# The opening of a three-layer kernel: another order of all queues, with more of the weight preparation on GpSimd

## The chip, the cores and the metric

One core of one Trainium2 chip runs the whole program. The metric is the device time of one execution in microseconds (us); a figure without more is the median of several executions. The engines are TensorE (PE) for matrix products, VectorE (DVE), ScalarE (ACT), GpSimd (POOL), and SyncE (SP), which here issues the DMAs. They run side by side, each through its own queue of instructions in a fixed order, and meet at semaphores.

## What is computed

Attention over a window of 128 positions, whose result goes through two feed-forward layers:

```python
# _attn_ref: batch 4, 8 heads, 576 positions, head size 64
scores = scale * np.matmul(q, k.transpose(0, 1, 3, 2))
bias = slopes[:, None, None] * (-np.abs(rel).astype(np.float32))[None, :, :]
mask = (rel >= 0) & (rel < window)
scores = np.where(mask, scores + bias[None], -1000000000.0)
attn = np.exp(scores - max); attn = attn / (sum + 1e-09)
x = np.matmul(attn, v)                       # 2304 tokens x 512
# _moe_ref: 512 -> 1024 -> 512
h = x @ w_in
solu = h * softmax(h)
ln = (solu - mu) / np.sqrt(var + 1e-06) * g_ln
x = ln @ w_out
# _moe2_ref: 512 -> 1536 -> 512
g = x @ w_gate
out = (g * (1.0 / (1.0 + np.exp(-g))) * (x @ w_val)) @ w_out2
```

All in float32. The large products split each factor into a high and a low part and run three fast passes: high x high, high x low, low x high.

## The kernel before

**Tiles.** The 2304 tokens are 18 tiles of 128. For each tile t the heads come in two groups g of four. The first two layers are one loop over the tiles (`step`), three stages deep; the third layer (`period`, `out_product`) follows and is not touched. Tiles 0 to 2 and the scores of tile 3 have their own, hand-written order in each of the five queues: the functions `opening()`. After them every queue goes on with `step(3)`, whose first work on PE is `qk_scores(4, 0)` (L558).

**A tile's way.** SP loads keys and queries (`load_early` for tiles 1 to 3, `load_qk` from 4 on) and v. PE makes scores (`early_scores(a, g)`, L545). ACT copies the half that belongs to the previous tile's keys into `fold` (`copy_prev`), DVE puts the own half over it (`select_own`, L1120) and finds the maxima (`find_max`). ACT takes the exponentials (`exp_scores`, L837 and L840), DVE inverts the sums (`invert_sums`, L1134), and POOL scales `fold` (`scale_probs`, L1467; DVE does it for tile 0). PE transposes (`transpose_probs`, L567), DVE masks (`unfold`, L1153), PE multiplies with v (`attend`, L582). ACT and DVE split the result (`x_hi_part`, `x_lo_part`). PE makes the hidden layer in two halves n of four chunks c (`hidden(t, n, odd, chunks)`, L596). DVE finds its maximum (`max_hidden`), ACT the exponentials (`exp_hidden`), DVE the product and the statistics (`make_solu`, `find_stats`, `scale_variance`), POOL the factor (`find_factor`, L1472 to L1478), ACT normalises. PE transposes (`transpose_ln`, L609), ACT and DVE split (`ln_hi`, `ln_lo`). `layer1_out` (L623) multiplies with w_out for two tiles at a time.

**The weight pieces.** Eight pieces of 128x1024 (512 KB) go through four buffers `stage`: pieces 0 to 3 are w_in (chunk c of `hidden(0, 0)` waits for the low part of piece c), pieces 4 to 7 are w_out. `load_piece(n)` for n of 4 and more waits for the low part of piece n - 4. A piece is split in two steps: the high part is a copy (ACT, L813), the low part a difference (`piece` on POOL, L1506 for w_in and L1512 for w_out, or on DVE, L1205). The rows of w_out are also scaled by the norm weights g_ln first, in two instructions of 512 columns: on ACT (L889) for pieces 4, 6 and 7, on POOL (`gain_piece`, L1461) for piece 5, as `POOL_GAINS` says. Before, the low parts of w_in are POOL's for pieces 0 and 1 and DVE's for 2 and 3. POOL also makes the low parts of the keys (`split_last_k`, L1445, for tile 3, and `split_qk`, L1434 and L1437, two instructions for each group) and copies rows of positions (`put_positions`, L1451).

**Fillers.** `keep_warm(n)` (L524) issues n products of 128x128 whose result nobody reads.

**Order.** Nothing reorders the queues: a queue whose head waits holds all behind it. `scores_ready`, `x_ready`, `probs_ready` and so on count the units done, so `wait_ge(scores_ready, 2 * (t - 1) + g + 1)` in `load_early` holds SP, and all loads behind, until PE has made the scores that free the buffer.

## Time and profile before

| | us |
|---|---|
| median of 3 runs | 721.79 (721.65 to 722.07) |
| the profiled execution | 720.79 |
| its span, first to last instruction | 719.0 |

Busy shares of the span: PE 99%, DVE 67%, ACT 57%, POOL 54%. The profile page splits the span into 40 slices and shows for each the busy tenths of the engines and the TensorE clock that was granted. The trace behind it is asked in views: the waits (who waited for whom), the timeline (instructions in order of time, equal ones in a row merged), groups of instructions by line and form, and DMA issues with the time to landing. In a row, `banks` is PSUM, `out<-in` names the tiles, and L with a number is a line of the kernel. The end of a matrix product is modelled, its start is measured.

### The profile page before, as it was taken

The page shows a single profiled execution, that of the slowest core. Times are in us where ns is not written, and L with a number is a line of the kernel's source. Part 1 is how long each engine was busy: PE and PEld are TensorE (multiplying, and loading weights), DVE is VectorE, ACT ScalarE, POOL GpSimd, SP SyncE. Part 2 cuts the span into 40 slices and gives each one's busy share as a digit, 9 for nine tenths or more (in the row PEclk, how much of TensorE's full clock was granted, in tenths as well). Part 3 has the DMA queues.
Part 4 walks back from the last instruction along what each step waited for, and adds up shares of the span by engine and source line. Part 5 has one row for each costly group of instructions (what it writes and reads, how often), then busy time and mean ns, then how long its engine had stood idle before and what let it go on. Part 6 is the DMA issues. An engine that isn't in the chain of part 4 may idle for free.

```text
span 719.0 us, 13230 instructions
## 1 busy us (share of the span) xinstructions
PE 711.5 (99%) x4732; PEld 682.6 (95%) x4732; DVE 482.4 (67%) x851; ACT 412.3 (57%) x843; POOL 390.3 (54%) x398
## 2 busy tenths in 40 slices
PE   8999999999999999999999999999999999999998
PEld 7779999999999999999999999999999999999998
DVE  5987777777777777747976555655556699754650
ACT  6997777777777776673634443344433487245340
POOL 3785444444445555894838958769576937300000
PEclk9999999999999999999999999999999999999999
DMA  8734443333333323134223432414336765795822
GB/s 326 285 104 162 166 143 120 129 134 128 117 117 117 117 73 118 33 115 132 84 101 135 153 107 107 150 64 154 107 107 242 256 234 190 274 375 191 283 75 88
DMA packets 49197, 109.85 MB, mean 153 GB/s; under 512 B 3841, under 2 KB 30209, under 8 KB 49153
## 3 DMA queue, kind: packets, MB, share of 16 engines
q1 hardware_dynamic: 49152, 109.27, 43.5%
q8 instruction: 27, 0.44, 0.2%
q14 instruction: 18, 0.14, 0.1%
HBM read 75.04 MB, written 34.21 MB: 152 GB/s over the span
## 4 chain that ended last, share of the span: by engine, by line
PE 95%; DVE 2%; DMA 2%; issue 0%; SPq 0%; ACT 0%; DVEq 0%
PE banks L637 36%; PE banks L795 18%; PE banks L623 15%; PE banks L596 13%; PE banks L582 4%; PE banks L609 2%; PE banks L567 2%; PE banks L558 2%; PE banks L559 2%; DMA early<-in_early 1%; DMA v<-in_v 1%; PE banks L545 1%; DVE win_lo L1205 0%; DVE xs_lo L1213 0%; DVE fold L1120 0%
## 5 line engine op out<-in xcount | busy, mean ns | idle before, releaser
L637 PE MATMUL banks<-xs_hi,w_hi 128*128 128x384 f32 x504 | 169.5, 336 | 0.1
L637 PE MATMUL banks<-xs_hi,w_lo 128*128 128x384 f32 x504 | 169.3, 336 | 0.0
L637 PE MATMUL banks<-xs_lo,w_hi 128*128 128x384 f32 x504 | 169.1, 336 | 0.0
L637 PEld LDWEIGHTS banks<-xs_hi,w_hi 128*128 128x128 f32 x504 | 94.7, 188 | 0.7 <-DVE xs_lo L1213 0.4
L637 PEld LDWEIGHTS banks<-xs_lo,w_hi 128*128 128x128 f32 x504 | 94.7, 188 | 0.0
L637 PEld LDWEIGHTS banks<-xs_hi,w_lo 128*128 128x128 f32 x504 | 94.7, 188 | 0.0
L623 PE MATMUL banks<-lnt_hi,wout_hi 128*128 (+1 forms) x288 | 85.5, 297 | 0.0
L795 PE MATMUL banks<-lot_hi,wo_hi 128*128 128x384 f32 x252 | 84.8, 337 | 0.1
L795 PE MATMUL banks<-lot_hi,wo_lo 128*128 128x384 f32 x252 | 84.5, 335 | 0.0
L795 PE MATMUL banks<-lot_lo,wo_hi 128*128 128x384 f32 x252 | 84.4, 335 | 0.0
L813 ACT ACTIVATE g_sum<-banks 128x384 f32<-128x384 f32 x84 | 41.2, 490 | 72.1 <-PE banks L637 55.9
L623 PE MATMUL banks<-lnt_lo,wout_hi 128*128 (+1 forms) x288 | 81.4, 283 | 0.0
L623 PE MATMUL banks<-lnt_hi,wout_lo 128*128 (+1 forms) x288 | 81.4, 283 | 0.0
L1236 DVE TENSOR_TENSOR lot_lo<-lot_raw,lot_hi 128x768 fp32r<-128x768 f32 x63 | 61.7, 1036 | 22.4 <-ACT lot_hi L813 22.4
L1434 POOL TENSOR_TENSOR k_lo<-qk_raw,kq 64x512 fp32r<-64x512 f32 x28 | 36.0, 1286 | 58.9 <-ACT kq L813 58.9
L1522 POOL TENSOR_TENSOR w_raw<-w_raw 128x256 f32<-128x256 f32 x48 | 41.1, 856 | 46.4 <-DMA w_raw<-in_wb 43.5
L1549 POOL TENSOR_TENSOR w_lo<-w_raw,w_hi 128x256 fp32r<-128x256 f32 x77 | 65.3, 883 | 0.8 <-ACT w_hi L813 0.8
L1467 POOL TENSOR_TENSOR fold<-fold,pinv 128x512 f32<-128x512 f32 x34 | 35.4, 1042 | 44.0 <-DVE pinv L1136 44.0
L596 PE MATMUL banks<-win_hi,xt_hi 128*128 128x512 f32 x144 | 56.9, 395 | 1.2 <-DVE xt_lo L1160 1.1
L813 ACT ACTIVATE lot_hi<-lot_raw 128x768 fp32r<-128x768 f32 x63 | 48.1, 834 | 17.4 <-DMA lot_raw<-unit_scratch 17.4
L1241 DVE TENSOR_TENSOR g_sum<-banks,g_sum 128x384 f32<-128x384 f32 x42 | 23.3, 556 | 51.1 <-PE banks L637 45.2
L623 PEld LDWEIGHTS banks<-lnt_hi,wout_hi 128*128 128x128 f32 x288 | 55.0, 191 | 2.6 <-issue 2.6
(106 smaller groups left out, 1751.5 us busy)
## 6 DMA issues: line engine op xcount, KB each, us to landing
lot_raw<-unit_scratch SPq DMA_DIRECT2D x63, 384.0 KB, 5.6
qk_raw<-in_qk SPq DMA_DIRECT2D x28, 768.0 KB, 4.2
unit_scratch<-st_sums SPq DMA_DIRECT2D x18, 576.0 KB, 4.7
unit_scratch<-st_even SPq DMA_DIRECT2D x18, 384.0 KB, 2.5
unit_scratch<-st_odd SPq DMA_DIRECT2D x18, 384.0 KB, 3.2
w_raw<-in_wb SPq DMA_DIRECT2D x12, 512.0 KB, 4.6
v<-in_v SPq DMA_DIRECT2D x18, 256.0 KB, 2.6
x_scratch<-x_out SPq DMA_DIRECT2D x18, 256.0 KB, 2.6
```

What stands on the lines that cost most here:

```text
L582: last = mm(ps_x[HD * half:HD * (half + 1), c * P:(c + 1) * P], v[:, of_v, head * HD:(head + 1) * HD], of_p[:, g, 2 * pair + half, :], sta ...
L596: last = mm(ps_h[:, n, :], xt[l][:, odd, c, :], win[r][:, c, n * 512:(n + 1) * 512], start=c == 0 and k == 0, stop=c == CM - 1 and k == 2)
L623: last = mm(ps, wout1[l][:, c, f * P:(f + 1) * P], lnt[r][:, gx % 2, c, :], start=c == 0 and n == 0, stop=c == C1 - 1 and n == 2)
L637: last = mm(ps[n % 2], w_of[l][:, k * P:(k + 1) * P], x_of[r][:, k * HALF:(k + 1) * HALF], start=start and k == 0 and i == 0, stop=k == 1 ...
L795: last = mm(ps[p], w_of[l][:, c, p * P:(p + 1) * P], lot_parts[lot % RING][r][:, cols], start=start and c == 0 and i == 0, stop=c == CHUNK ...
L813: return nc.scalar.activation(out, in_, ACT.Copy)
L1236: nc.vector.tensor_tensor(lo[:, :], lot_raw[k % RING][:, :], hi[:, :], ALU.subtract).then_inc(lot_done, 1)
L1241: nc.vector.tensor_tensor(g_sum[n % 2][:, 1, :], ps_c[n % 2], g_sum[n % 2][:, 1, :], ALU.add).then_inc(gates_done, 1)
L1434: nc.gpsimd.tensor_tensor(k_lo[k, g, :, odd, :], qk_raw[k, g, :, 2 * odd, :], kq[k, g, :, 3 * odd, :], ALU.subtract).then_inc(k_lo_done, 1)
L1467: nc.gpsimd.tensor_tensor(fold[:, g, :, :], fold[:, g, :, :], inv, ALU.mult).then_inc(probs_ready, 1)
L1522: last = nc.gpsimd.tensor_tensor(out[:, cols], one[:, cols], two[:, cols], op)
L1549: last = nc.gpsimd.tensor_tensor(w_parts[b][1][:, slot, :], w_raw[b][:, slot, :], w_parts[b][0][:, slot - 1, :], ALU.subtract)
```

## The change

Only the openings change, and what they need:

- POOL makes the high part of piece 1 (`piece_hi`, with a semaphore of its own, `win_hi_pool`), which was ACT's. `win_hi_of(n)` says whose semaphore counts piece n.
- The low parts of w_in: DVE takes pieces 0 and 2, POOL 1 and 3.
- POOL scales pieces 6 and 7 instead of 5, ACT 4 and 5 instead of 4, 6 and 7.
- `keep_warm(2)` ahead of `transpose_probs(0, 0)`, and 6 instead of 4 fillers ahead of `attend(0, 0)`.
- All five queues have another order. On SP, `early(2,0)` stands ahead of v(0), the last keys of tile 3 ahead of piece 2; v(1) is earlier, piece 7 and `qk(4,1)` later. On PE, `early_scores(2, 1)` and `(3, 0)` are earlier, `(3, 1)` is behind `attend(2, 0)`, and `hidden` is cut so that transposes come in between.

The diff, without most of its unchanged lines:

```diff
--- before.py
+++ after.py
@@ -73,7 +73,7 @@
...
 E_MASK, E_SLOTS = 8, 17
-POOL_GAINS = (5,)
+POOL_GAINS = (6, 7,)
 ACT_GAINS = tuple(n for n in range(CM, 8) if n not in POOL_GAINS)
@@ -193,6 +193,7 @@
...
         warm_set = sem("warm_set")
+        win_hi_pool = sem("win_hi_pool")
         win_hi, win_lo_pool, win_lo_dve = sem("win_hi"), sem("win_lo_pool"), sem("win_lo_dve")
@@ -262,9 +263,14 @@
...
+        def win_hi_of(n):
+
+            pool_takes = (1,)
+            return (win_hi_pool if n in pool_takes else win_hi), 1 + sum((m in pool_takes) == (n in pool_takes) for m in range(n))
+
         def win_lo(n):
-            return (win_lo_pool, win_lo_pool, win_lo_dve, win_lo_dve)[n], (1, 2, 1, 2)[n]
+            return (win_lo_dve, win_lo_pool, win_lo_dve, win_lo_pool)[n], (1, 1, 2, 2)[n]
@@ -361,24 +367,24 @@
...
                 load_piece(1)
+                load_early(2, 0)
                 load_v(0, 0)
-                load_piece(2)
-                load_early(2, 0)
-                load_piece(3)
-                load_piece(4)
-                load_early(2, 1)
-                load_piece(5)
                 for g in range(2):
                     load_last_k(g)
+                load_piece(2)
+                load_piece(3)
+                load_early(2, 1)
+                load_v(1, 1)
+                load_piece(4)
+                load_early(3, 0)
+                load_piece(5)
                 load_piece(6)
-                load_v(1, 1)
-                load_early(3, 0)
-                load_piece(7)
                 load_early(3, 1)
...
                 load_v(2, 0)
+                load_piece(7)
+                load_v(3, 1)
                 load_qk(4, 1)
-                load_v(3, 1)
                 for g in range(2):
@@ -725,33 +731,41 @@
...
                 pe.wait_ge(const_in, 16)
+                keep_warm(2)
                 transpose_probs(0, 0)
...
                 transpose_probs(0, 1)
-                keep_warm(4)
+                keep_warm(6)
                 attend(0, 0)
...
                 transpose_probs(1, 0)
-                hidden(0, 0, 0, range(1, CM))
-                hidden(0, 1, 0)
+                hidden(0, 0, 0, range(1, 3))
+                early_scores(2, 1)
+                hidden(0, 0, 0, range(3, CM))
+                hidden(0, 1, 0, range(0, 1))
                 transpose_probs(1, 1)
-                early_scores(2, 1)
+                hidden(0, 1, 0, range(1, CM))
                 attend(1, 1)
+                early_scores(3, 0)
                 transpose_probs(2, 0)
-                early_scores(3, 0)
                 hidden(1, 0, 1)
-                hidden(1, 1, 1)
+                hidden(1, 1, 1, range(0, 2))
+                transpose_probs(2, 1)
+                hidden(1, 1, 1, range(2, CM))
                 transpose_ln(0, 0, 0)
-                transpose_probs(2, 1)
+                attend(2, 0)
                 early_scores(3, 1)
-                attend(2, 0)
+                hidden(2, 0, 0, range(0, 1))
+                hidden(2, 0, 0, range(1, 3))
                 transpose_ln(0, 1, 0)
-                hidden(2, 0, 0)
+                hidden(2, 0, 0, range(3, CM))
+                hidden(2, 1, 0, range(0, 1))
                 transpose_probs(3, 0)
+                hidden(2, 1, 0, range(1, 2))
                 transpose_ln(1, 0, 1)
-                hidden(2, 1, 0)
+                hidden(2, 1, 0, range(2, CM))
                 transpose_ln(1, 1, 1)
@@ -996,35 +1010,34 @@
...
                 exp_scores(0, 1)
+                copy_prev(1, 0, 1)
                 piece(0)
-                copy_prev(1, 0, 1)
-                piece(1)
                 copy_prev(1, 1, 1)
...
                 piece(3)
+                copy_prev(2, 0, 0)
                 exp_scores(1, 1)
-                copy_prev(2, 0, 0)
-                piece(4)
                 exp_scores(2, 0)
                 split_last_k(0)
+                split_last_k(1)
                 copy_prev(2, 1, 0)
+                piece(4)
                 exp_hidden(0, 0)
-                piece(5)
                 x_hi_part(1, 1)
                 exp_scores(2, 1)
+                piece(5)
                 copy_prev(3, 0, 1)
-                split_last_k(1)
                 piece(6)
...
                 split_qk(4, 0, 0)
+                ln_hi(0, 0, 0, 0)
                 exp_hidden(1, 1)
-                ln_hi(0, 0, 0, 0)
+                x_hi_part(2, 0)
+                piece(7)
                 exp_scores(3, 0)
                 copy_prev(3, 1, 1)
-                x_hi_part(2, 0)
-                piece(7)
                 ln_hi(0, 1, 0, 0)
@@ -1201,7 +1214,7 @@
...
-                dve.wait_ge(win_hi, n + 1)
+                dve.wait_ge(*win_hi_of(n))
                 nc.vector.tensor_tensor(win[1][:, n, :], stage[:, n % STAGES, :], win[0][:, n, :],
@@ -1322,43 +1335,43 @@
...
                 select_own(1, 1, 1)
-                find_max(1, 1)
+                piece(0)
                 invert_sums(1, 0)
                 x_lo_part(0, 0)
+                find_max(1, 1)
                 piece(2)
-                piece(3)
-                invert_sums(1, 1)
                 select_own(2, 0, 0)
                 find_max(2, 0)
+                invert_sums(1, 1)
                 unfold(1, 0)
+                invert_sums(2, 0)
                 max_hidden(0, 0, 0)
                 unfold(1, 1)
+                select_own(2, 1, 0)
                 max_hidden(0, 1, 0)
-                invert_sums(2, 0)
-                select_own(2, 1, 0)
                 find_max(2, 1)
...
                 find_stats(0, 0)
+                invert_sums(2, 1)
                 scale_variance(0, 0)
-                invert_sums(2, 1)
+                unfold(2, 0)
                 select_own(3, 0, 1)
-                unfold(2, 0)
                 max_hidden(1, 0, 1)
+                unfold(2, 1)
+                max_hidden(1, 1, 1)
                 find_max(3, 0)
-                max_hidden(1, 1, 1)
-                unfold(2, 1)
+                ln_lo(0, 0, 0, 0)
                 make_solu(1, 1)
-                ln_lo(0, 0, 0, 0)
+                x_lo_part(2, 0)
                 find_stats(1, 1)
-                x_lo_part(2, 0)
                 scale_variance(1, 1)
...
                 find_max(3, 1)
+                max_hidden(2, 0, 0)
                 ln_lo(0, 1, 0, 0)
                 unfold(3, 0)
-                max_hidden(2, 0, 0)
                 invert_sums(3, 1)
@@ -1461,6 +1474,11 @@
...
+            def piece_hi(n):
+                pool.wait_ge(stage_in[n % STAGES], 16)
+                nc.gpsimd.tensor_copy(win[0][:, n, :], stage[:, n % STAGES, :]).then_inc(win_hi_pool, 1)
+                pool.wait_ge(*win_hi_of(n))
+
             def scale_probs(t, g):
@@ -1502,7 +1520,7 @@
...
                 if n < CM:
-                    pool.wait_ge(win_hi, n + 1)
+                    pool.wait_ge(*win_hi_of(n))
                     nc.gpsimd.tensor_tensor(win[1][:, n, :], src, win[0][:, n, :],
@@ -1582,26 +1600,28 @@
...
                 pool.wait_ge(const_in, 16)
-                piece(0)
+                piece_hi(1)
                 piece(1)
                 scale_probs(1, 0)
+                piece(3)
                 scale_probs(1, 1)
-                gain_piece(5)
-                pool.wait_ge(probs_ready, 4)
-                put_positions(0)
                 scale_probs(2, 0)
                 split_last_k(0)
+                pool.wait_ge(probs_ready, 5)
+                put_positions(0)
+                split_last_k(1)
+                gain_piece(6)
                 piece(4)
+                scale_probs(2, 1)
                 find_factor(0, 0)
-                scale_probs(2, 1)
+                gain_piece(7)
+                piece(5)
+                split_qk(4, 0, 0)
                 pool.wait_ge(probs_ready, 6)
                 put_positions(1)
-                piece(5)
-                split_last_k(1)
-                piece(6)
                 find_factor(1, 1)
                 scale_probs(3, 0)
-                split_qk(4, 0, 0)
+                piece(6)
                 scale_probs(3, 1)
...
                 split_qk(4, 1, 0)
```

## Rows read from the trace of the kernel before

**Rows 1.** page, parts 1 and 2: busy time, granted TensorE clock by slices

```profile
PE 711.5 (99%) x4732; PEld 682.6 (95%) x4732; DVE 482.4 (67%) x851; ACT 412.3 (57%) x843; POOL 390.3 (54%) x398
...
PEclk9999999999999999999999999999999999999999
```

**Rows 2.** waits of PE in 0 to 60 us: us in total, times, longest

```profile
PE banks L545 <- DMA early<-in_early: 1.6, 2, 1.2
PE banks L596 <- DVE xt_lo L1160: 1.1, 1, 1.1
```

**Rows 3.** timeline of PE: start us, duration, line, operation, [idle before, releaser]

```profile
13.66 1.06 PE L524 MATMUL banks<-solu 128*128 128x128 f32 x8
14.65 0.66 PE L582 MATMUL banks<-p_own,v 128*64 128x128 f32 x8
...
18.59 0.47 PE L596 MATMUL banks<-win_hi,xt_hi 128*128 128x512 f32 x1 [0.15 <-issue]
...
46.16 0.60 PE L567 MATMUL banks<-const,fold 128*128 128x128 f32 x4
...
50.63 0.36 PE L558 MATMUL banks<-kq 128*128 128x256 f32 x1
```

**Rows 4.** timeline of SP's issues: start us, duration of issuing

```profile
4.15 0.51 SPq L346 DMA_DIRECT2D v<-in_v  x1
4.71 0.95 SPq L351 DMA_DIRECT2D stage<-in_wa  x1
11.25 0.33 SPq L329 DMA_DIRECT2D early<-in_early  x1
...
18.07 1.54 SPq L338 DMA_DIRECT2D qk_raw<-in_qk  x2
```

**Rows 5.** DMA issues near 4.2, 4.7, 15.8, 18.1, 41.7 us; last: to landing

```profile
v<-in_v SPq DMA_DIRECT2D x1, 256.0 KB, 9.5
...
stage<-in_wa SPq DMA_DIRECT2D x1, 512.0 KB, 10.3
...
stage<-in_wa SPq DMA_DIRECT2D x1, 512.0 KB, 5.3
...
qk_raw<-in_qk SPq DMA_DIRECT2D x1, 256.0 KB, 6.0
...
v<-in_v SPq DMA_DIRECT2D x1, 256.0 KB, 3.4
```

**Rows 6.** timeline of ACT

```profile
17.11 1.99 ACT L813 ACTIVATE win_hi<-stage 128x1024 fp32r<-128x1024 f32 x2
...
23.59 0.19 ACT L837 ACTIVATE scaled<-negmax 128x4 f32<-128x4 f32 x1
...
25.36 0.62 ACT L813 ACTIVATE kq<-qk_raw 128x512 fp32r<-128x512 f32 x1
```

**Rows 7.** timeline of POOL

```profile
28.16 1.04 POOL L1467 TENSOR_TENSOR fold<-fold,pinv 128x512 f32<-128x512 f32 x1 [0.39 <-DVE pinv L1136]
...
43.76 0.56 POOL L1472 TENSOR_TENSOR rstd<-var,const 128x1 f32<-128x1 f32 x1 [1.11 <-DVE var L1194]
...
44.81 1.04 POOL L1467 TENSOR_TENSOR fold<-fold,pinv 128x512 f32<-128x512 f32 x1
```

**Rows 8.** POOL by form, 0 to 54 us: busy us, mean ns, idle before

```profile
L1512 POOL TENSOR_TENSOR wout_lo<-stage,wout_hi 128x1024 fp32r<-128x1024 f32 x4 | 9.5, 2382 | 0.2
L1467 POOL TENSOR_TENSOR fold<-fold,pinv 128x512 f32<-128x512 f32 x6 | 6.3, 1042 | 3.9 <-DVE pinv L1136 3.9
...
L1461 POOL TENSOR_SCALAR stage<-stage,const 128x512 f32<-128x512 f32 x2 | 3.1, 1571 | 0.9 <-DMA stage<-in_wa 0.8
L1437 POOL TENSOR_TENSOR kq<-qk_raw,kq 64x512 fp32r<-64x512 f32 x2 | 2.6, 1302 | 0.2
...
L1445 POOL TENSOR_TENSOR k_lo<-qk_raw,kq 64x512 fp32r<-64x512 f32 x2 | 2.6, 1283 | 0.0
L1451 POOL CAST k_lo<-const 64x1024 fp32r<-64x1024 f32 x2 | 2.1, 1038 | 0.1
```

## The prediction

> **What bounds the kernel now.** I read the page first: TensorE (PE) is busy nearly all of the span, and its granted clock is full in all 40 slices [rows 1]. Then the waits of PE. In the first 60 us the largest sums are 1.6 us for `early` tiles and 1.1 us for `xt_lo` [rows 2]; the same view of 54 to 719 us has no line. So behind the opening PE never waits, and the change, which touches only the opening, can do one thing: move the moment at which PE starts `qk_scores(4, 0)`, the first work of the loop, now at 50.63 us [rows 3]. Whatever it moves, the end moves by as much. Therefore the third view is the timeline of PE in the opening (what starts when), and then those of SP's issues, of ScalarE (ACT) and of GpSimd (POOL), since these set when PE may start.
>
> PE itself does the same products before and after, plus four fillers. The sum is thus: new start of the loop = old start + fillers that don't fall into a wait + waits added - waits removed. For the waits I walked the five queues of the opening in their written order, old and new, with the durations of the trace: each operation starts when its engine is free and what it waits for is done.
>
> **Fillers.** Two are added ahead of `transpose_probs(0, 0)`, two more ahead of `attend(0, 0)`. Four took 13.66 to 14.65 us [rows 3], 0.25 us each, so 1.0 us for four. The first two delay the transposes and with them the chain on VectorE (DVE) by 0.5 us at most; the other two fall into a wait that the change itself makes (next part). All 1.0 us delays `attend(0, 0)` only if v is there.
>
> **The loads.** Before, v(0) and piece 2 are issued at 4.15 and 4.71 us, ahead of `early(2,0)`, which waits for scores and goes out at 11.25 [rows 4]; they land 9.5 and 10.3 us later, at 13.65 and 15.0 [rows 5]. After, `early(2,0)` stands in front of both, so SP holds v(0) until 11.25 + 0.4 = 11.6 us, and behind it come both last-k loads, then pieces 2 and 3. From an empty queue v of 256 KB took 3.4 us [rows 5]. The pieces queued one behind the other land some 1.3 us apart for 512 KB (the 256 KB of v 0.7 us), so the fixed part is 3.4 - 0.7 = 2.7 us. Walked on: `early(2,0)` 15.2, v(0) 15.9, last k 16.6 and 17.3, piece 2 18.7, piece 3 20.0 us. The nearest row that speaks for later is a piece issued around 16 us that took 5.3 us [rows 5], 1.3 us more than 2.7 + 1.3; it is the upper bound. The lower one is that all land as before.
>
> **What hangs on them.** `attend(0, 0)` starts at 14.65 now, after at 15.95 (0.9 us from the fillers and their start, 0.4 us waiting for v), and `hidden(0, 0)` at 18.7 in the walk, hardly later than the 18.59 of now [rows 3], since ACT and DVE are then free for the split. ACT splits pieces 2 and 3 from 17.11 in one go, at 1.0 us each [rows 6]; after, it has them only at 18.7 and 20.0, so it leaves piece 3 at 21.0. Behind the waiting `piece(3)` on ACT stand `copy_prev(2, 0)`, `exp_scores(1, 1)` and `exp_scores(2, 0)`. The copy costs 0.5 us, an `exp_scores` 1.8 us (23.59 to 25.36 [rows 6]), so `exp_scores(2, 0)` ends at 25.1 and `invert_sums(2, 0)` lets POOL scale at 25.6 us. (Before this is at 28.16 [rows 7], late because DVE does `invert_sums(2, 0)` behind `unfold(1, 1)` and `max_hidden(0, 1)`; that is a real gain of the new order, 2.5 us for POOL.) PE's waits from this part: 0.8 us for the low part of piece 2 ahead of chunk 2 of `hidden(0, 0)` (0.5 us before, ahead of chunk 3), 0.4 us at `early_scores(2, 1)`, which needs `select_own(2, 0)` and so that copy.
>
> **POOL.** ACT gives up the high part of piece 1 (1.0 us) and a net one of its three scalings (1.3 us). ACT isn't last, so this buys nothing by itself. POOL gets the high part, a cast of 128x1024. The trace has only a cast of 64x1024 at 1.04 us [rows 8]; by lanes it could be anything from that to double; I take 1.04, the same elements per partition. It lies ahead of 18 us, where POOL then waits 1.4 us for `inv_ready`, so at up to double it costs nothing; with less cover it costs itself. The second scaling counts: POOL scales two pieces where it scaled one, 2 x 1.57 us more [rows 8], and between `scale_probs(2, 0)` and `scale_probs(3, 0)` it now does: 3 `scale_probs` 3.1, 2 `split_last_k` 2.6, 2 `put_positions` 2.1, 4 scaling instructions 6.3, 2 low parts of w_out 4.8, `split_qk(4, 0)` 2.6, 2 `find_factor` 2.1 (43.76 to 44.81 [rows 7]): 23.6 us, with gaps of some hundredths 23.8. All inputs are there in time, so it runs from 25.6 to 49.4 without a pause. Before, the scaling of piece 5 lay ahead of `scale_probs(2, 0)`, in a stretch where POOL had been waiting, and `scale_probs(3, 0)` ended at 45.85 [rows 7].
>
> The Trainium skill, "GPSIMD Engine Reference" (4.1, engine selection), says otherwise of such an instruction: with one tensor as input GpSimd runs at roughly line rate, and only two inputs make it slow. The cast, which has one input, shows what that would be: 1024 elements in 1.04 us, so a scaling instruction of 512 in 0.52 us and four of them 4.2 us less. For the scaling the trace doesn't agree: 1.57 us, more than the 1.04 us of the two-input product of the same size [rows 8]. The row decides, and what the rule would give is rival 1.
>
> **PE behind POOL.** `transpose_probs(3, 0)` waits for `scale_probs(3, 0)`; it starts at 46.16 now [rows 3] and 49.5 after. Other waits on POOL's delays: `transpose_probs(2, 1)` 0.7 (scaling of piece 6 and a low part stand ahead of its `scale_probs`), `transpose_ln(0, 0)` 0.5 (`find_factor(0, 0)` ends at 38.0, was 34.4), and `hidden(2, 0)` 0.8 where it was 1.1 [rows 2]. `transpose_probs(3, 0)` itself waits 1.5. From there to the loop: its own 0.44, three chunks of `hidden(2, 1)` at 0.69, two `transpose_ln` and `transpose_probs(3, 1)` at 0.44, 0.3 waiting: 4.1 us (4.5 now, with one chunk more). So the loop starts at 53.6.
>
> Waits after, in sum: 0.4 + 0.8 + 0.4 + 0.2 + 0.7 + 0.5 + 0.8 + 1.5 + 0.3 = 5.6 us, against 3.0 us of the same walk through the old order, plus 1.0 us of fillers: 3.6 us. The walk through the old order gives 50.05 us for the loop's start where the trace has 50.63, so the difference to the trace is 3.0 us. I take the middle, **3.3 us slower**. Of SP's moves only one more matters: `qk(4,1)` now stands behind v(3), which waits for `attend(2, 0)`; issued at 42.3 instead of 40.2 it lands near 47, and ACT wants it at 51.9: no cost.
>
> The profiled execution took 720.8 us (span 719.0), the median of the runs is 721.8, 1.0 us more. So 720.8 + 3.3 = 724.1 profiled, 725.1 as a median. Bounds of this case: loads landing as before take 1.3 us off (2.0 slower, 723.8), landing 1.3 us later adds 1.1, and the gap of 0.3 on either side: up to 4.8 slower, 726.6.
>
> **Rivals.**
> 1. POOL doesn't decide. For: only two scaling instructions stand in the trace [rows 8], side by side, and spans on POOL are rough. If all four ran at the rate of the cast, 0.52 us each, `scale_probs(3, 0)` would end near 45.5, the low parts and `find_factor` would come in time, and the walk gives 2.9 us less (not 4.2, as 0.4 us stays at `transpose_probs(3, 0)`, behind ACT and DVE): 0.4 slower, 722.2, within what can be told from no change. Against: these two instructions started 1.6 us apart. 0.14.
> 2. Faster: the waits shown are what the new order takes away. The 1.1 us ahead of `hidden(2, 0)` goes since `attend(2, 0)`, `early_scores(3, 1)` and the ln transpose are spread, and the 2.5 us that POOL starts earlier outweigh the scaling. All 3.0 us of waits gone less 1.0 us of fillers: 719.8. It decides if piece 3 lands before 18 us and POOL is through with `scale_probs(3, 0)` by 45 us, that is in 20 us where the rows sum to 23.6. 0.08.
> 3. The loads collide worse: v(0), last k and both pieces, now issued within 2.5 us, share the 16 engines instead of following one another (a 256 KB load of last k amid others took 6.0 us where v alone took 3.4 [rows 5]), so that v lands near 18 and piece 3 near 22: 2 us on top, 727.1. 0.06.
> The forecast keeps 0.72.
>
> **How the numbers follow.** A measurement of this kernel can tell about 0.2%, 1.4 us, from no change: faster is below 720.4, slower above 723.2. Slower: 0.72 + 0.06, less a little for the low edge of the main case and rival 1 spilling both ways: 0.77. Same: 0.15. Faster: 0.08. The range goes from rival 1 (722.2) to 727.0, between the upper bound and rival 3; outside are rival 2, half of rival 3 and some of rival 1.
>
> **What would show each step.** v(0) issued at 11.6 and landing near 16, piece 3 landing near 20; ACT idle ahead of `win_hi` twice around 18 to 20 us; four `TENSOR_SCALAR` on POOL at 1.57 us each after 30 us; POOL without a pause from 25.6 to 49; PE waiting for POOL's `fold` ahead of `transpose_probs(2, 1)` and (3, 0), the latter starting at 49.5; PE's first `kq` product near 53.6 instead of 50.63; no waits behind it. I am wrong if POOL has pauses ahead of 45 us, or if pieces land at their old times.

## The result and the profile after

| | before | after |
|---|---|---|
| median, us | 721.25 (720.17 to 722.07, 6 runs) | 725.33 (724.09 to 725.62, 6 runs) |
| the profiled execution, us | 720.79 | 724.99 |
| its span, us | 719.0 | 723.2 |
| first `kq` product of PE (start of the loop), us | 50.63 | 54.82 |

The ratio is 1.0057, 95% interval 1.0045 to 1.0068: 4.1 us slower. Of some 140 executions behind all the ratios below, two are left out: one of e2 that took 742.05 us at a mean granted clock of 0.914, and one of e5 that took 2501.95 us. All of it lies ahead of the loop: from the loop's first product to the end of the span it is 668.4 us in both.

The waits of PE in the first 60 us, after (us in total, times, longest), against [rows 2]:

```profile
PE banks L573 <- DVE p_prev L1167: 1.4, 1, 1.4
PE banks L573 <- POOL fold L1485: 1.3, 1, 1.3
PE banks L588 <- DMA v<-in_v: 1.1, 1, 1.1
...
PE banks L551 <- DMA early<-in_early: 0.7, 1, 0.7
PE banks L551 <- DVE fold L1133: 0.4, 1, 0.4
PE banks L602 <- DVE win_lo L1218: 0.4, 1, 0.4
PE banks L602 <- DVE xt_lo L1173: 0.3, 1, 0.3
...
PE banks L615 <- DVE lnt_lo L1212: 0.2, 1, 0.2
```

Six of them are new: for v (L588), for two `transpose_probs` (L573), for `select_own` (L551, the `fold` line), and two short ones, for the low part of piece 2 (`win_lo`) and for `lnt_lo`. The 1.1 us for `xt_lo` of [rows 2] has shrunk to 0.3. Where they lie, in PE's timeline, against [rows 3]:

```profile
13.68 1.50 PE L530 MATMUL banks<-solu 128*128 128x128 f32 x12
16.33 1.09 PE L588 MATMUL banks<-p_own,v 128*64 128x128 f32 x16 [1.15 <-DMA v<-in_v]
...
19.00 0.58 PE L602 MATMUL banks<-win_hi,xt_hi 128*128 128x512 f32 x1
...
38.64 0.63 PE L573 MATMUL banks<-const,fold 128*128 128x128 f32 x4 [1.38 <-DVE p_prev L1167]
...
50.65 0.65 PE L573 MATMUL banks<-const,fold 128*128 128x128 f32 x4 [1.28 <-POOL fold L1485]
...
54.82 0.36 PE L564 MATMUL banks<-kq 128*128 128x256 f32 x1
```

The loads that come late, as the issues show them (near 11.3, 13.1 and 13.6 us; last: us to landing), against [rows 5]:

```profile
v<-in_v SPq DMA_DIRECT2D x1, 256.0 KB, 5.1
...
stage<-in_wa SPq DMA_DIRECT2D x1, 512.0 KB, 6.1
...
stage<-in_wa SPq DMA_DIRECT2D x1, 512.0 KB, 6.7
```

v(0) lands at 16.3, piece 2 at 19.1 and piece 3 at 20.4 us. ScalarE sits idle for both pieces, and `copy_prev(2, 0)` comes behind them, against [rows 6]:

```profile
19.19 1.06 ACT L827 ACTIVATE win_hi<-stage 128x1024 fp32r<-128x1024 f32 x1 [1.12 <-DMA stage<-in_wa]
20.47 1.06 ACT L827 ACTIVATE win_hi<-stage 128x1024 fp32r<-128x1024 f32 x1 [0.22 <-DMA stage<-in_wa]
21.43 0.58 ACT L827 ACTIVATE fold<-banks 128x512 f32<-128x512 f32 x1
```

POOL's cast of piece 1, and then POOL from `scale_probs(2, 0)` to `scale_probs(3, 0)`, against [rows 7] (the work on keys and positions from 27.06 to 30.90 and from 44.66 to 48.48 and the small instructions of `find_factor` are left out):

```profile
12.69 1.32 POOL L1479 CAST win_hi<-stage 128x1024 fp32r<-128x1024 f32 x1 [11.01 <-DMA stage<-in_wa]
...
26.06 1.04 POOL L1485 TENSOR_TENSOR fold<-fold,pinv 128x512 f32<-128x512 f32 x1 [0.73 <-DVE pinv L1149]
...
30.90 3.23 POOL L1474 TENSOR_SCALAR stage<-stage,const 128x512 f32<-128x512 f32 x2
34.21 2.41 POOL L1530 TENSOR_TENSOR wout_lo<-stage,wout_hi 128x1024 fp32r<-128x1024 f32 x1
36.94 1.04 POOL L1485 TENSOR_TENSOR fold<-fold,pinv 128x512 f32<-128x512 f32 x1 [0.32 <-DVE pinv L1149]
...
39.02 3.23 POOL L1474 TENSOR_SCALAR stage<-stage,const 128x512 f32<-128x512 f32 x2
42.33 2.37 POOL L1530 TENSOR_TENSOR wout_lo<-stage,wout_hi 128x1024 fp32r<-128x1024 f32 x1
...
49.55 1.04 POOL L1485 TENSOR_TENSOR fold<-fold,pinv 128x512 f32<-128x512 f32 x1
```

One pause of 0.32 us in 24.5 us. `transpose_probs(3, 0)` starts at 50.65, right behind it.

### The profile page after: what moved, and what is told of

It is laid out like the page before. It is cut to its first block, busy times and chain, and to the rows that moved or that the text cites. A ratio compares the mean times of both kernels' runs of the same rounds, so it can differ in the third digit from the quotient of the medians.

```text
span 723.2 us, 13248 instructions
## 1 busy us (share of the span) xinstructions
PE 713.1 (99%) x4740; PEld 683.7 (95%) x4740; DVE 483.4 (67%) x851; ACT 410.5 (57%) x840; POOL 394.4 (55%) x401
## 3 DMA queue, kind: packets, MB, share of 16 engines
HBM read 75.04 MB, written 34.21 MB: 151 GB/s over the span
## 4 chain that ended last, share of the span: by engine, by line
PE 92%; DMA 2%; DVE 2%; POOL 2%; ACT 1%; issue 1%; SPq 0%; POOLq 0%; DVEq 0%; ACTq 0%
PE banks L643 36%; PE banks L809 18%; PE banks L629 15%; PE banks L602 12%; PE banks L588 4%; PE banks L615 2%; PE banks L564 2%; PE banks L565 2%; PE banks L573 2%; DMA early<-in_early 1%; DMA stage<-in_wa 1%; PE banks L551 1%; POOL stage L1474 0%; DVE pden L1147 0%; POOL wout_lo L1530 0%
```

## The experiments

All ratios are to the kernel before, on the same chip in the same session; the sessions ran on several chips, and the intervals of two changed kernels often overlap, so a difference between two of them below some 1.4 us is not clear of noise by the ratios alone. e7 and e8 are one execution each, read for their profiles. "Loop" is the start of PE's first `kq` product in the profiled execution (50.63 before, 54.82 after). From there to the end each took 668.3 to 668.6 us (only e11 took 669.0, with one wait of 0.5 us behind the opening), so the loop's start and the time tell the same, apart from how a single execution's first loads land (some tenths, in two cases over a microsecond).

| run | edit | ratio (95%) | loop, us |
|---|---|---|---|
| after | | 1.0057 (1.0045 to 1.0068) | 54.82 |
| e1_scale_one_piece | POOL scales only piece 7 | 1.0027 (1.0016 to 1.0038) | 53.02 |
| e2_loads_early | v(0), pieces 2 and 3 early | 1.0040 (1.0024 to 1.0056) | 53.39 |
| e3_no_extra_fillers | without the four fillers | 1.0064 (1.0045 to 1.0083) | 54.02 |
| e4_add_by_columns | one addition as four | 1.0050 (1.0033 to 1.0067) | 53.97 |
| e5_both_undone | e1, e2 and e3 together | 1.0017 (1.0007 to 1.0026) | 52.31 |
| e10_high_part_on_act | cast back on ACT | 1.0047 (1.0031 to 1.0063) | 54.75 |
| e7_add_128x4_amid_pool | the addition put amid POOL's work | one execution, 725.2 us | 55.02 |
| e8_columns_amid_pool | the same, by columns | one execution, 723.9 us | 53.68 |
| e6_before_late_loads | before, SP order of after | 1.0042 (1.0026 to 1.0057) | 54.20 |
| e12_late_loads_8_fillers | e6 with four fillers more | 1.0035 (1.0023 to 1.0048) | 53.38 |
| e9_before_two_scalings | before, POOL scales 5 and 7 | 1.0029 (1.0017 to 1.0041) | 54.82 |
| e11_before_add_columns | before, one addition as four | 0.9989 (0.9978 to 0.9999) | 50.49 |

**The theories.** The prediction's: POOL has one scaling too many between `scale_probs(2, 0)` and `scale_probs(3, 0)`, and the late loads start that stretch late. Rivals: only one of the two matters; the fillers do; the order of the other queues does.

**POOL's scaling.**

```diff
-POOL_GAINS = (6, 7,)
+POOL_GAINS = (7,)
...
-                gain_piece(6)
                 piece(4)
```

> The changed kernel with GpSimd scaling only piece 7; ScalarE scales piece 6 (one POOL scaling, 3.2 us, less ahead of scale_probs(2, 1)). Theory (POOL decides the opening): scale_probs(3, 0) on POOL starts about 2 us earlier (49.55 in the changed kernel), the loop's first qk product at about 52.9 us instead of 54.82, time 1.9 us below the changed kernel. Rival (the late loads decide, POOL only fills waits): the first qk product stays within 0.4 us of 54.8. Second rival (ScalarE takes POOL's place as the last): under 1 us gained.

The loop starts at 53.02, `scale_probs(3, 0)` on POOL at 47.74. The time falls from 1.0057 to 1.0027, about 2.2 us. The two waits for POOL and for what follows it are gone from PE (L573 0.2 us in all), so ScalarE did not take POOL's place. VectorE did, in part: of the 3.3 us taken from POOL's work 1.8 came through at `scale_probs(3, 0)`, since POOL now stands 1.44 us for `pinv` ahead of `scale_probs(2, 1)` and 0.41 us for `var` ahead of `find_factor(1, 1)`. From the other side, the old kernel with the scaling of piece 7 on POOL as well:

```diff
-POOL_GAINS = (5,)
+POOL_GAINS = (5, 7)
...
                 put_positions(1)
+                gain_piece(7)
                 piece(5)
```

> The kernel before with one part of the change alone: GpSimd also scales piece 7 (behind the second put_positions, ahead of the low part of piece 5), ScalarE is relieved of it. Theory (POOL is near its limit in the opening even in the old order): POOL's scale_probs(3, 0) starts at about 47.0 instead of 44.81, transpose_probs(3, 0) waits 1.9 us for it, and the first qk product is at 52.5, 1.9 us slower. Rival (POOL's 6 us of idle time in the opening take it): under 0.5 us slower.

1.0029, 2.1 us slower, and PE waits 1.9 us for `fold`, once, as expected. The waits of PE in 0 to 60 us:

```profile
PE banks L545 <- DMA early<-in_early: 2.3, 2, 1.4
PE banks L567 <- POOL fold L1467: 1.9, 1, 1.9
```

The profiled execution was the slowest of the six (725.04, median 723.10), and its loop starts at 54.82 instead of the 52.5 expected. PE's timeline behind the wait shows most of it:

```profile
48.75 0.66 PE L567 MATMUL banks<-const,fold 128*128 128x128 f32 x4 [1.91 <-POOL fold L1467]
...
50.36 0.63 PE L596 MATMUL banks<-win_hi,xt_lo 128*128 128x512 f32 x1
50.79 0.63 PE L596 MATMUL banks<-win_hi,xt_hi 128*128 128x512 f32 x1
...
53.34 0.40 PE L596 MATMUL banks<-win_hi,xt_hi 128*128 128x512 f32 x1
53.57 0.40 PE L596 MATMUL banks<-win_lo,xt_hi 128*128 128x512 f32 x1
```

and the granted clock by stretches of 5 us (columns: PE busy, number, granted clock, DMA share, GB/s):

```profile
45.00:50.00 5.00, 3.09 (x18) 0.99 0.61 210
50.00:55.00 5.00, 5.00 (x21) 0.67 0.47 157
```

From 49.93 to 53.34 the products of 128x512 start 0.43 us apart and take 0.63; behind, and everywhere else, 0.23 us apart and 0.39. The granted clock is 0.67 in that stretch, where it is 1.00 in all others. At least eight of these intervals, 0.2 us longer each, are some 1.6 us. Another 0.7 us is waiting for `early` beyond [rows 2]. Without both the loop would start at 52.5.

**The loads.**

```diff
+                load_v(0, 0)
+                load_piece(2)
                 load_early(2, 0)
-                load_v(0, 0)
+                load_piece(3)
                 for g in range(2):
                     load_last_k(g)
-                load_piece(2)
-                load_piece(3)
```

> The changed kernel with v(0) and piece 2 issued ahead of early(2,0) and piece 3 right behind it, as in the kernel before; the rest of the SP order is that of the change. Theory (late loads and POOL add up): the wait for v(0) on PE (1.1 us) and ScalarE's wait for piece 2 (1.1 us) go, POOL's scale_probs(2, 0) starts 1.3 us earlier, and so does the first qk product: 53.5 us. Rival (POOL alone decides): the first qk product stays at 54.8, the waits on POOL grow by what the others lose.

53.39 and 1.0040, some 1.2 us less by the ratios, which is not clear of noise: the interval (1.0024 to 1.0056) overlaps that of the change (1.0045 to 1.0068). The wait for v and that for the low part of piece 2 are gone; `scale_probs(2, 0)` starts at 24.90 (26.06), the one of tile 3 at 48.10 (49.55). So 1.2 of the 1.4 us that the profile gained are there when POOL's stretch starts. The other 0.3 us are chance, as the part on VectorE's addition shows: it did not wait here. The start itself varies from one execution to the next with the landing of the loads: in the seven profiles that keep the change's order on SP (after, e1, e3, e4, e7, e8, e10) it lies between 25.27 and 26.27, all later than the 24.90 of e2. In the old kernel, with SP's opening taken whole from the change, so with more moved than e2 moves back:

> The kernel before with only the change's order of SP's loads in the opening; all other queues are those of before. Theory (late loads cost by themselves): v(0) lands near 16.3 us, PE waits for it 1.5 to 2 us ahead of attend(0, 0), pieces 2 and 3 come to ScalarE at 19.2 and 20.5 and hold exp_scores(1, 1) behind them, transpose_probs(2, 0) waits over 1 us more; the first qk product at 53.2 us instead of 50.63, 2.6 us slower. Rival (late loads are covered, only POOL matters): under 0.7 us slower.

The waits of PE in 0 to 60 us:

```profile
PE banks L582 <- DMA v<-in_v: 2.0, 1, 2.0
PE banks L567 <- POOL fold L1467: 1.4, 1, 1.4
PE banks L596 <- DVE xt_lo L1160: 1.1, 1, 1.1
```

1.0042, 3.0 us slower, with 2.0 us of waiting for v and 1.4 for `fold`. So the change's order of loads costs more in the old kernel (3.0) than the three loads that e2 moves back cost in the new one (1.2). The two edits are not the same, and the difference is about as large as the intervals leave open. Two things in the profile could be why. One is the clock, which fell again behind the long wait; PE's timeline:

```profile
16.81 1.94 PE L582 MATMUL banks<-p_own,v 128*64 128x128 f32 x16 [1.99 <-DMA v<-in_v]
18.68 2.77 PE L545 MATMUL banks<-early 128*128 128x256 f32 x8
```

```profile
10.00:15.00 5.00, 4.83 (x30) 1.00 0.79 287
15.00:20.00 5.00, 3.19 (x19) 0.69 1.02 360
```

The same two groups took 1.09 and 1.99 us in the profile after: 1.6 us. The other is POOL, which scales piece 5 in the old kernel and has to wait for it; its timeline:

```profile
27.31 3.23 POOL L1461 TENSOR_SCALAR stage<-stage,const 128x512 f32<-128x512 f32 x2 [2.07 <-DMA stage<-in_wa]
...
31.73 1.04 POOL L1467 TENSOR_TENSOR fold<-fold,pinv 128x512 f32<-128x512 f32 x1
```

`scale_probs(2, 0)` at 31.73 is 3.6 us behind the 28.16 of [rows 7]. To take the long wait away and leave the loads late, e12 has `keep_warm(8)` where e6 has `keep_warm(4)`, ahead of `attend(0, 0)`.

> e6_before_late_loads (the old kernel with the SP order of the change) with eight fillers instead of four ahead of attend(0, 0). In e6's profile TensorE stood 1.99 us for v at 16.81, and behind that the granted clock of 15 to 20 us was 0.69: the 16 products of attend took 1.94 us and the eight of early_scores(2, 0) 2.77, against 1.09 and 1.99 in the changed kernel, where six fillers leave a wait of 1.15 us and the clock stays at 1.00. Theory (the length of the wait ahead decides the clock, and the lower clock is about 1.5 us of the 3.0 that the late loads cost): four fillers more take about 1.0 us out of the wait (it becomes 0.9 to 1.1), v lands no sooner, the two groups take 1.1 and 2.0 us, the granted clock of 15 to 20 us is 1.00, the loop starts near 52.7 (e6 54.20), and the ratio is 1.002 to 1.003 (e6 1.0042). Rival (the clock has another cause, or what it costs is waited away at fold anyway): the wait shrinks, the loop starts at 54.0 to 54.4 and the ratio stays at 1.004 to 1.0045.

PE's timeline, and then POOL's:

```profile
13.86 1.95 PE L524 MATMUL banks<-solu 128*128 128x128 f32 x16
15.74 1.09 PE L582 MATMUL banks<-p_own,v 128*64 128x128 f32 x16
16.76 1.99 PE L545 MATMUL banks<-early 128*128 128x256 f32 x8
```

```profile
26.52 3.23 POOL L1461 TENSOR_SCALAR stage<-stage,const 128x512 f32<-128x512 f32 x2 [1.70 <-DMA stage<-in_wa]
...
30.95 1.04 POOL L1467 TENSOR_TENSOR fold<-fold,pinv 128x512 f32<-128x512 f32 x1
```

The wait for v is gone, more than the 1.0 us of four fillers can explain: v landed 4.0 us after its issue here and 5.2 us in e6, where "v lands no sooner" was expected. The groups take 1.09 and 1.99 us again, and the clock is 1.00 in all stretches. Yet the loop starts at 53.38, in the middle between the two expectations, and the ratio of 1.0035 can't be told from e6's. What settles it is that three of e6's four executions had a mean granted clock of 1.000 and took 724.02 to 724.40, no less than the profiled one (724.38, 0.998). So the clock isn't what the late loads cost in the old order: my theory for e12 fell. What is the same in e6 and e12 is POOL: piece 5 comes at 26.5 or 27.3, and `scale_probs(2, 0)` is 2.8 or 3.6 us late; the loop is 2.75 and 3.57 us late in the same two profiles. That the one makes the other is read off the profiles; no run tried it by itself. In the changed kernel POOL scales pieces 6 and 7 instead, behind `scale_probs(2, 0)`, and doesn't stand in that wait.

**The fillers.** `keep_warm(2)` removed, the other back from 6 to 4.

> The changed kernel without the four added fillers (none ahead of transpose_probs(0, 0), four ahead of attend(0, 0)). Theory: they stand in waits that the loads make, so PE's wait for v(0) grows from 1.1 to 2.1 us and the first qk product stays at 54.8 within 0.3. Rival (the fillers are on the path): 1.0 us earlier, 53.8. Rival (they keep the clock up): products behind the longer wait take longer, and it comes later than 54.8.

1.0064, whose interval takes in the change itself, but by itself hardly excludes the 1.0 us of the first rival. The profile's 54.02 is 0.8 us earlier, for two other reasons: v and the pieces happened to land 0.5 to 0.8 us earlier in it (PE stood only 0.5 us for v, not the 2.1 expected), and VectorE's addition did not wait (next point). e4, which has all the fillers, shows that it is these: its POOL starts `scale_probs(2, 0)` at 25.56 where e3's starts at 25.59, its addition doesn't wait either, and its loop starts at 53.97.

**VectorE's addition.** In the profile after, one small instruction stands out in VectorE's timeline, beside POOL's difference of 34.21 (shown above):

```profile
34.28 2.37 DVE L1147 TENSOR_SCALAR pden<-psumrow 128x4 f32<-128x4 f32 x1
```

The addition of 1e-9 to 128x4 sums took 2.37 us and ended as POOL's difference did (36.65 and 36.62). `unfold(2, 0)` stands behind it, and `transpose_probs(2, 1)` waits for that: 1.38 us. In e3 the same addition came 0.07 us behind POOL's start, as here, and took 0.12 us. So the edits also decided, by tenths, whether this happened: in e2 too it took 0.12 us, and in e1 it fell where POOL was idle. In e4 it was made by columns in this one unit:

```diff
-                nc.vector.tensor_scalar_add(pden[:, g, :], psumrow[:, g, :], 1e-9).then_inc(den_ready, 1)
+                if is_at(t, 2) and g == 1:
+                    for h in range(4):
+                        last = nc.vector.tensor_scalar_add(pden[:, g, h:h + 1], psumrow[:, g, h:h + 1], 1e-9)
+                    last.then_inc(den_ready, 1)
...
```

> In the changed kernel, VectorE's addition of 1e-9 to 128x4 sums in invert_sums(2, 1) took 2.37 us instead of 0.17, ending as POOL's difference of w_out did. Here this one addition is made as four of 128x1; all else is the same. Theory (this form of VectorE instruction waits until a running GpSimd instruction ends, the 128x1 form doesn't, since those in find_stats ran beside POOL in 0.15 us): the four take 0.3 to 0.6 us in all, PE's wait ahead of transpose_probs(2, 1) falls from 1.38 to about 0.7 us, and the first qk product comes 0.4 us earlier at 54.4 (POOL is last behind it anyway). Rival (the 2.37 us is a late semaphore or operand): the first of the four takes about 2.2 us and nothing moves.

0.28 us, loop at 53.97, and the ratio of 1.0050 can't be told from that of the change. But this addition too began next to POOL's start, so it doesn't tell the form from chance. Two more kernels do: one `bn_stats` more ahead of it, into a tile that nobody reads, puts it amid POOL's instruction.

```diff
+                if is_at(t, 0):
+                    nc.vector.bn_stats(unused[:, :], solu[:, odd, 0:512])
...
```

> The changed kernel with one more bn_stats of 512 elements on VectorE, into a tile nobody reads, ahead of find_stats(0): this puts the addition of 1e-9 to 128x4 sums in invert_sums(2, 1) 0.6 us later, surely amid POOL's 2.4 us difference of w_out instead of at its very start. Theory (the 128x4 form waits for the end of a running POOL instruction): the addition takes 1 to 2 us and ends when POOL's instruction ends. Rival (the 2.37 us seen was a late operand): 0.17 us.

> As e7_add_128x4_amid_pool, but the addition in invert_sums(2, 1) is made as four of 128x1 (as in e4). Theory (only the form with several elements per partition waits for POOL): the four take 0.3 us in all amid POOL's instruction. Rival (any such VectorE instruction waits): the first takes 1 to 2 us.

With 128x4, VectorE's timeline and then POOL's:

```profile
35.07 1.78 DVE L1148 TENSOR_SCALAR pden<-psumrow 128x4 f32<-128x4 f32 x1
```

```profile
34.41 2.41 POOL L1533 TENSOR_TENSOR wout_lo<-stage,wout_hi 128x1024 fp32r<-128x1024 f32 x1
```

With four of 128x1 (the reciprocal of 128x4 behind them did not wait either), VectorE's and POOL's:

```profile
34.08 0.28 DVE L1150 TENSOR_SCALAR pden<-psumrow 128x1 f32<-128x1 f32 x4
34.39 0.18 DVE L1155 RECIPROCAL pinv<-pden 128x4 f32<-128x4 f32 x1
```

```profile
33.42 2.40 POOL L1538 TENSOR_TENSOR wout_lo<-stage,wout_hi 128x1024 fp32r<-128x1024 f32 x1
```

The first ends at 36.85, POOL at 36.82; the second takes 0.28 us in the middle of POOL's 2.40. Beside this instruction the form decides. The price is smaller than the 0.8 us between the loops of 54.8 and 54.0, as POOL's timeline in e4 shows beside that of the change (26.06 and 49.55):

```profile
25.56 1.04 POOL L1490 TENSOR_TENSOR fold<-fold,pinv 128x512 f32<-128x512 f32 x1 [0.73 <-DVE pinv L1154]
...
48.70 1.04 POOL L1490 TENSOR_TENSOR fold<-fold,pinv 128x512 f32<-128x512 f32 x1
```

| profile | the addition, us | `scale_probs(2, 0)` starts | `scale_probs(3, 0)` starts | between them | loop |
|---|---|---|---|---|---|
| after | 2.37 | 26.06 | 49.55 | 23.49 | 54.82 |
| e10 | 2.03 | 25.96 | 49.48 | 23.52 | 54.75 |
| e7 | 1.78 | 26.27 | 49.74 | 23.47 | 55.02 |
| e2 | 0.12 | 24.90 | 48.10 | 23.20 | 53.39 |
| e3 | 0.12 | 25.59 | 48.75 | 23.16 | 54.02 |
| e4 | 0.28 | 25.56 | 48.70 | 23.14 | 53.97 |
| e8 | 0.28 | 25.27 | 48.41 | 23.14 | 53.68 |

With the wait POOL stands 0.32 us for `pinv` ahead of `scale_probs(2, 1)`, and its stretch is 0.3 us longer; the rest of the difference is there at its start already and comes from the loads. The loop starts 5.3 us behind `scale_probs(3, 0)` in all seven. So the addition costs 0.3 us when it waits, near the 0.4 us that was expected for e4.

The old kernel has such a wait too, 0.94 us at 16.76 in `invert_sums(1, 0)`; the same edit for that unit:

> The kernel before, whose addition to 128x4 sums in invert_sums(1, 0) took 0.94 us and ended with POOL's win_lo, made as four of 128x1 for this unit alone. Theory: it takes 0.3 us, x_lo_part(0, 0) ends up to 0.5 us earlier and so does the start of hidden(0, 0), 18.59 before; but the low part of piece 3 and later hidden(2, 0) wait for VectorE anyway, so the first qk product is 0 to 0.4 us earlier than 50.63 and the time the same. Rival (VectorE's chain is the path all through the opening): 0.6 us earlier.

Loop at 50.49, ratio 0.9989 (0.9978 to 0.9999): 0.8 us, or 0.1%, at the edge of what can be told, and the only kernel here that is not behind the old one. The addition took 0.34 us as four. In its profile the loop gained only 0.14 us, so that more than this comes from the edit is not shown.

**The cast.** The high part of piece 1 back on ScalarE.

> The changed kernel with the high part of piece 1 back on ScalarE, behind that of piece 0; all else is the same. Theory (the 1.3 us cast on GpSimd lies ahead of 18 us, where POOL then waits 1.4 us for inv_ready): POOL's scale_probs(1, 0) still starts near 18.0, the first qk product stays within 0.3 us of 54.8, or of 54.0 if VectorE's 128x4 addition in invert_sums(2, 1) happens not to wait for POOL. Rival (the cast is a part of the loss): over 0.7 us earlier than that. Rival (ScalarE's copy holds copy_prev(1, 1) and costs more): later than 55.3.

54.75, and the ratio within the interval of the change. `scale_probs(1, 0)` on POOL still starts at 18.40. The cast took 1.32 us in the profile after and cost nothing that can be told.

**Both undone.**

> The changed kernel with GpSimd scaling only piece 7 (as e1), v(0) and piece 2 issued ahead of early(2,0) and piece 3 right behind it (as e2), and without the four added fillers (as e3). Theory (one scaling too many on POOL and late loads are the whole loss): the two gains add, the first qk product comes at 50.8 to 51.6 us, near the 50.63 of the kernel before, and the time is 0 to 1.2 us above the kernel before. Rival (the order of PE, ScalarE and VectorE costs by itself): 52.5 us or later, 2 us above the kernel before. Rival (with its two burdens gone the new order is better): below 50.3 us.

1.0017 (1.0007 to 1.0026), 1.2 us slower than before: the upper end of what the theory gave for the time. Its profiled loop start of 52.31 is nearer to the rival's 52.5, but it holds a start that was 0.8 us later than in the profile after (PE's first score product at 5.01 instead of 4.23 us). So the burdens, with the fillers, are 2.9 of the 4.1 us, and the new order without them is still about 1.2 us behind. In this profile PE needs 36.14 us from `attend(0, 0)` (16.17) to the loop, against 35.98 us before (from 14.65), so what this execution lost lies ahead of `attend(0, 0)`: the late start, and 0.42 us of waiting for VectorE's `fold` ahead of `transpose_probs(0, 1)`. Which moves of the new order make the 1.2 us of the medians stays open: the five orders fit each other, and no run exchanged one of them alone except SP's.

## Why the prediction was right

725.1 was forecast, 3.3 us slower; 725.33 came, 4.1 us slower.

- **Nothing behind the opening.** Right: 668.4 us from the loop's start to the end, before and after.
- **The loads.** v(0) at 15.9, pieces at 18.7 and 20.0 were forecast; 16.3, 19.1 and 20.4 came. The order of magnitude of the fixed part was right, each 0.4 us late. `hidden(0, 0)` started at 19.00 (18.7). e6 and e12 show that the change's order of loads costs, 3.0 and 2.5 us in the old kernel; the 1.2 us of e2 in the new one are seen at POOL's start but are not clear of noise in the time.
- **The fillers.** Right that they lie in the wait for v: without them the loop starts where e4's does with them (54.02 and 53.97).
- **The cast.** Taken at 1.04, measured 1.32 us; hidden, as forecast (e10).
- **POOL.** The stretch from `scale_probs(2, 0)` began at 26.06 (25.6) and took 24.5 us (23.8); the scaling instructions took 1.57 us again. `transpose_probs(3, 0)` waited 1.3 us (1.5) and started at 50.65 (49.5). e1 and e9 show 2.2 and 2.1 us for one scaling; 1.9 was expected for each. The sign "I am wrong if POOL has pauses ahead of 45 us" came true by the letter, with one pause of 0.32 us at 36.6; as the sum shows, it doesn't overturn the path.
- **The mis-sized terms.** The path to the loop was right: POOL's start, POOL's stretch, and PE behind it, forecast at 25.6 + 23.8 + 0.1 + 4.1 = 53.6. Of the 1.2 us up to the measured 54.82, 0.5 us is the later start, from the loads. 0.7 us is the stretch, 24.5 instead of 23.8: 0.3 us of it is the pause that VectorE's addition made (the walk gave an addition of 128x4 its usual 0.17 us wherever it fell), 0.1 us the instructions themselves (23.7 in sum, not 23.6), and 0.3 us the gaps between them.
- **The wait ahead of `transpose_probs(2, 1)`** had the wrong cause: 0.7 us forecast for POOL, 1.38 measured, for VectorE. It cost PE nothing by the loop's start, since POOL releases `transpose_probs(3, 0)` later anyway. The 0.5 us forecast ahead of `transpose_ln(0, 0)` did not come.
- **A little luck.** The walk gave 3.6 us from its own old order and 3.0 from the trace, and the forecast took the middle. That doesn't rest on a mechanism; 4.1 came.
- **Rival 1**, POOL not deciding: fell with e1 and e9. The rule beside it, of the Trainium skill ("GPSIMD Engine Reference", 4.1), GpSimd at roughly line rate with one input, does not hold for these instructions: 1568 ns for 512 elements in the mean of four.
- **Rival 2**, faster: the wait for `xt_lo` did shrink by 0.8 us, as it said, and POOL did start 2.1 us earlier at `scale_probs(2, 0)`. Both were paid back by the second scaling.
- **Rival 3**, loads colliding worse: v at 16.3 instead of 18. It did not come.

What stays open is the 1.2 us of e5.

## What to carry to other kernels

Where the main engine never waits behind a prologue, all of a change there is the start of the loop: sum the work of each helper engine between the two points where it is last, and look whether it fits. An engine with idle time in sum can still be full in the one stretch that decides: POOL was idle for some 6 us of the old opening, and one scaling of 3.2 us more cost 2.1. A load that doesn't depend on the wait ahead of it in a queue should be issued ahead of that wait. And a small operation of VectorE on the path may not be small beside a long one of GpSimd: 2.37 instead of 0.17 us here, of which 0.3 us reached the loop.

## What the hardware showed that was not expected

VectorE's addition of a constant to 128x4 elements in SBUF, 0.12 to 0.18 us alone, mostly waits for the end of a GpSimd instruction that runs already: 2.37, 2.03 (in e10) and 1.78 us, each ending within 0.1 us of POOL's. With 128x1 elements it doesn't (0.28 us for four), nor does the reciprocal of 128x4 (0.18). When POOL's instruction started 0.07 us ahead, it came out either way: 2.37 us in one run, 0.12 in another. The old profile had it as well: 0.94 us at 16.76. In e12 it waited 0.49 us for the end of POOL's second scaling instruction. There is one clear exception in these profiles, in e6, amid the same instruction of POOL (28.98 to 30.55 us there):

```profile
29.84 0.16 DVE L1134 TENSOR_SCALAR pden<-psumrow 128x4 f32<-128x4 f32 x1
```

The Trainium skill gives a reason for the wait, in "SBUF — State Buffer" ("Who interferes with whom"): VectorE and GpSimd share one pair of SBUF ports as an exclusive lock, held for a whole instruction by whoever comes first, and `tensor_scalar` can be in a mode that needs it. These runs agree with that where the addition came clearly later and waited; the exception in e6 doesn't follow from it. The page also says that it is the order of issue that decides who waits; with starts 0.07 us apart no run here shows that order. What the page's conditions on the operands are for 128x1 against 128x4, no run here shows beyond this pair of forms.

The granted clock of PE fell for a few microseconds in two of the profiled executions, from 1.00 (2.4 GHz) to 0.67 and 0.69 of it in a stretch of 5 us, with products 0.43 us apart instead of 0.23, so near the lower level of 1.2 GHz there. Both times PE had just stood for the longest single waits of all these profiles, 1.91 us in e9 and 1.99 in e6; in the other profiles no single wait in the opening was over 1.4 us, and the clock was 1.00 throughout. It cost 1.6 us of PE's time where it happened. That the wait is the cause isn't shown: three executions of e6 had no drop in their mean clock, and what they waited for isn't on record. Over all kernels here, eight of some 140 executions had a mean granted clock of 0.997 or 0.998, and they took 0.3 to 2.2 us longer than the median of the others of their kernel in the same session (e5: 724.04 against 722.00; e12: 725.36 and 725.57 against 723.96). So a part of the scatter goes with the clock, in the two profiles that show it within the opening, and a profiled execution should be looked at for it before its loop start is compared. The view of the granted clock doesn't show everything: in every profile the first twelve filler products took 2.93 us and the same twelve later 1.50 (1.67 in e5), though it reads 1.00 in both stretches.
